# A fused attention and expert kernel: three tiles a turn, logits and turning in 64x64 blocks two tiles back, tile loads in halves

## The reference, cut to what matters

```python
def _attn_ref(q, k, v):
    scores = scale * np.matmul(q, k.transpose(0, 1, 3, 2))
    gamma = 1.0 - 2.0 ** (-5.0 - np.arange(H, dtype=np.float32))
    rel = pos[:, None] - pos[None, :]
    Dmat = np.where(rel >= 0, gamma[:, None, None] ** rel[None, :, :], 0.0)
    return np.matmul(scores * Dmat[None, :, :, :], v)

def _moe_ref(x, phi, w1, w2):
    logits = x @ phi
    d = softmax of logits over the tokens (axis 0)
    slot_input = d.T @ x
    for e in range(E):
        slot_out[e] = np.maximum(slot_input[e] @ w1[e], 0.0) @ w2[e]
    c = softmax of logits over the slots (axis 1)
    return c @ slot_out

def _moe2_ref(x, w1, w2, w3, w_out):
    return ((x @ w1) * (x @ w2) @ w3) @ w_out
```

## Time and profile before

| | |
|---|---|
| median of 3 runs | 394.13 us (391.75 to 395.69) |
| the profiled execution | 394.4 us, span 392.6 us |
| PE busy | 358.9 us, 91% of the span |
| DVE, ACT, POOL busy | 43%, 32%, 41% |
| DMA | 104.77 MB, mean 267 GB/s |
| the tile loop | to about 166 us |

### The profile page before, as it was taken

The page is one execution under the profiler, slowest core; times in us unless marked ns, Lnnn a source line. Parts: engine busy times, 40 slices in busy tenths (PEclk is TensorE's granted clock), DMA queues, the critical chain, the costliest instruction groups (busy, mean ns, idle before and its releaser), DMA issues. The chain is left out here.

```text
span 392.6 us, 16090 instructions
## 1 busy us (share of the span) xinstructions
PE 358.9 (91%) x7123; PEld 278.2 (71%) x7123; DVE 167.5 (43%) x329; ACT 125.2 (32%) x275; POOL 161.9 (41%) x155
## 2 busy tenths in 40 slices
PE   2683987898999999999999999899999999999996
PEld 1573876777878887774656555468878888888885
DVE  1321454556757765573013000699853323233320
ACT  1000121321433342222324220532734444434442
POOL 2521222322443542133546451298954554554530
PEclk9856799999999999999999999999999999999999
DMA  7898499897887886879999996057226655556222
GB/s 262 351 387 341 149 398 426 337 374 250 312 308 240 313 310 231 314 294 411 427 425 427 425 428 273 0 92 237 76 88 228 230 189 188 190 179 235 114 107 107
DMA packets 25914, 104.77 MB, mean 267 GB/s; under 512 B 2660, under 2 KB 5284, under 8 KB 16164
## 3 DMA queue, kind: packets, MB, share of 16 engines
q1 hardware_dynamic: 25892, 104.47, 71.1%
HBM read 94.14 MB, written 10.32 MB: 266 GB/s over the span
## 5 line engine op out<-in xcount | busy, mean ns | idle before, releaser
L561 POOL TENSOR_TENSOR pkg_sb<-pkg_sb,const_sb 128x512 f32<-128x512 f32 x36 | 37.5, 1042 | 106.4 <-DMA pkg_sb<-in_tiles 106.4
L623 POOL TENSOR_TENSOR feat<-c_sb 128x512 f32<-128x512 f32 x45 | 56.9, 1275 | 46.2 <-PE psum L991 44.3
L991 PE MATMUL psum<-m_hi,feat_hi 128*128 128x512 f32 x144 | 56.1, 390 | 0.3 <-DVE m_lo L1480 0.3
L991 PE MATMUL psum<-m_lo,feat_hi 128*128 128x512 f32 x144 | 56.0, 389 | 0.0
L991 PE MATMUL psum<-m_hi,feat_lo 128*128 128x512 f32 x144 | 56.0, 389 | 0.0
L428 DVE TENSOR_TENSOR feat_lo<-feat,feat_hi 128x512 fp32r<-128x512 f32 x34 | 27.2, 801 | 62.2 <-ACT feat_hi L1149 61.0
L1249 DVE TENSOR_TENSOR x_t<-psum,x_decay 128x512 f32<-128x512 f32 x36 | 24.9, 691 | 40.9 <-PE psum L693 40.9
L1007 ACT COPY x_nat<-psum 128x512 f32<-128x512 f32 x36 | 21.1, 586 | 65.8 <-PE psum L705 65.8
L648 PE MATMUL psum<-pkg_sb 64*64 64x64 f32 x1152 | 26.9, 234 | 16.2 <-POOL pkg_sb L561 7.3
L693 PE MATMUL psum<-weights_t,pkg_sb 64*64 64x64 f32 x1152 | 35.3, 238 | 5.7 <-issue 5.5
L1149 ACT CAST feat_hi<-feat 128x512 fp32r<-128x512 f32 x45 | 27.9, 623 | 39.0 <-POOL feat L623 39.0
(11 more groups left out here) (138 smaller groups left out, 569.0 us busy)
## 6 DMA issues: line engine op xcount, KB each, us to landing
pkg_sb<-in_tiles SPq DMA_DIRECT2D x34, 1024.0 KB, 4.9
unit_a<-in_units SPq DMA_DIRECT2D x16, 1024.0 KB, 13.8
c_sb<-c_rows SPq DMA_DIRECT2D x45, 256.0 KB
unit_x<-in_units SPq DMA_DIRECT2D x9, 1024.0 KB, 14.1
out<-out_sb SPq DMA_DIRECT2D x36, 256.0 KB, 2.0
fold_raw<-in_fold SPq DMA_DIRECT2D x6, 1024.0 KB, 9.3
unit_y<-in_units SPq DMA_DIRECT2D x5, 1024.0 KB, 12.3
unit_n<-in_units SPq DMA_DIRECT2D x4, 1024.0 KB, 12.2
```

What stands on the lines that cost most here:

```text
L561: nc.gpsimd.tensor_tensor(v_nat(n).rearrange("p (h d) -> p h d", h=HEADS), v_nat(n).rearrange("p (h d) -> p h d", h=HEADS), decay.unsqueez ...
L623: nc.gpsimd.tensor_tensor(feat[:, k, :], c_sb[:, s, x, :], c_sb[:, s, y, :], ALU.mult).then_inc(feat_ready, 1)
L991: last = mm(psum[:, OUT + b, :], x, y, start=(at == 0 and m == 0), stop=(at == 4 and m == 2))
```

## The change

The loop now has three steps in its body and twelve turns. The parts:

- Tiles load in halves: turned k and q (`load_q_k`), plain k and v (`load_k_v`). The ring has three places. A q half is asked for when `through_states` has used the place (`q_used`), a v half when `update` has. POOL writes scaled v to `v_sb`, in three places of its own, and passes on that the q half is there (`pass_q_k`).
- The fold loads go behind tiles 4 to 7; of the first units two go out with no wait.
- Logits and turning take `x_t` in 64x64 blocks as the stationary side; the turning is a matmul with the identity. The two heads of a pair give separate sums of the logits in two banks, which DVE adds (`add_parts`) and turns. Both are of tile n - 2, and share two banks: logits wait until the turned tile before is copied (`x_copied`), turning waits until the logits are (`logits_copied`).
- The order in a step: logits of n - 2, update of n + 1, turning of n - 2, states, first pass, a dispatch where due, scores of n + 1, second pass. `weights_t` has one place, `x_t` three, `state_sb` six (so `states_used` goes).
- `shift_combine` and `divide_combine` of the first three groups go to POOL.
- Behind the loop, a logits and a turning of tile 34 and of tile 35 stand in turn with fold work.

```diff
-SLOTS_IN = 4
-STATES_IN = 4
+SLOTS_IN = 3
+STATES_IN = 6
...
-FOLD_AT = (10, 11, 14, 15)
+FOLD_AT = (4, 5, 6, 7)
...
+        v_sb = place("v_sb", [P, SLOTS_IN, D])
+        weights_t = place("weights_t", [P, 2, D // 2])
+        x_t = place("x_t", [P, SLOTS_IN, PAIRS, P])
...
+            def load_q_k(n):
 
                 if n >= SLOTS_IN:
 
-                    sp.wait_ge(out_ready, QUARTERS * (n - SLOTS_IN + 1))
-                sp.dma_start(tile_sb(n), pkg[n].rearrange("(p c) -> p c", p=P)).then_inc(tile_loaded[place_of(n)], 16)
+                    sp.wait_ge(q_used, QUARTERS * (n - SLOTS_IN + 1))
+                sp.dma_start(tile_sb(n)[:, 0:2 * D], pkg[n].rearrange("(p c) -> p c", p=P)[:, 0:2 * D]
+                             ).then_inc(q_k_loaded[place_of(n)], 16)
+
+            def load_k_v(n):
+
+                if n >= SLOTS_IN:
+
+                    for i in range(2):
+                        sp.wait_ge(update_ready[i], 2 * (n - SLOTS_IN + 1))
+                sp.dma_start(tile_sb(n)[:, 2 * D:4 * D], pkg[n].rearrange("(p c) -> p c", p=P)[:, 2 * D:4 * D]
+                             ).then_inc(k_v_loaded[place_of(n)], 16)
...
+            load_q_k(0)
+            load_k_v(0)
+            load_k_v(1)
+            load_q_k(1)
...
+            load_k_v(2)
+            load_q_k(2)
             load_first_unit(0)
+            load_first_unit(1)
+            load_k_v(SLOTS_IN)
+            load_first_unit(2)
             for n in range(SLOTS_IN, NTILES):
-                load_tile(n)
-                if n < SLOTS_IN + 2:
-                    load_first_unit(2 * n - 7)
-                    load_first_unit(2 * n - 6)
-                elif n == 8:
+                if n < NTILES - 1:
+                    load_k_v(n + 1)
+                load_q_k(n)
+                if n == SLOTS_IN:
+                    load_first_unit(3)
+                    load_first_unit(4)
+                elif n == SLOTS_IN + 1:
                     load_first_unit(5)
-                elif n in FOLD_AT:
+                if n in FOLD_AT:
...
-                    sp.wait_ge(out_ready, QUARTERS * (NTILES - 3 + (u - 6)))
+                    sp.wait_ge(out_ready, QUARTERS * (NTILES - 2 + (u - 6)))
...
+                pool.wait_ge(k_v_loaded[place_of(n)], (n // SLOTS_IN + 1) * 16)
+                if n >= SLOTS_IN:
+
+                    pool.wait_ge(out_ready, QUARTERS * (n - SLOTS_IN + 1))
                 decay = const_sb[:, C_VDECAY + HEADS * t:C_VDECAY + HEADS * (t + 1)]
                 nc.gpsimd.tensor_tensor(v_nat(n).rearrange("p (h d) -> p h d", h=HEADS),
-                                        v_nat(n).rearrange("p (h d) -> p h d", h=HEADS),
+                                        v_raw(n).rearrange("p (h d) -> p h d", h=HEADS),
                                         decay.unsqueeze(2).to_broadcast([P, HEADS, HD]),
                                         ALU.mult).then_inc(v_ready, 1)
+
+            def pass_q_k(n):
+
+                pool.wait_ge(q_k_loaded[place_of(n)], (n // SLOTS_IN + 1) * 16)
+                pool.sem_inc(q_k_ready, 1)
...
+            pass_q_k(0)
             for n in range(NTILES):
                 scale_v(n)
+                if n > 1:
+                    pass_q_k(n - 1)
                 if 1 <= n <= SEAM:
                     later_decay(n)
+                if n >= TILES + 2:
+                    g, t = divmod(n - 2, TILES)
+                    if t == 3:
+                        shift_combine(nc.gpsimd, pool, g - 1)
+                    if t == 8:
+                        divide_combine(nc.gpsimd, pool, g - 1)
...
+            def turn_x(r, consumes=True):
                 for a in range(PAIRS):
-                    last = nc.tensor.transpose(psum[:, X_NAT, P * a:P * (a + 1)], x_t[:, r % 2, a, :], ident)
-                last.then_inc(x_turned, 1)
-
-            def logits(r):
+                    for odd in range(2):
+                        rows = slice(HD * odd, HD * (odd + 1))
+                        for half in range(2):
+                            cols = slice(HD * half, HD * (half + 1))
+                            last = mm(psum[cols, X_NAT + odd, HD * a:HD * (a + 1)], x_t[rows, r, a, cols],
+                                      ident[rows, rows], start=True, stop=True)
+                            if (a, odd, half) == (0, 0, 0) and consumes:
+                                last.then_inc(logits_copied, -1)
+                            if a == PAIRS - 1:
+                                last.then_inc(x_turned, 1)
...
+            def logits(r, consumes=True):
                 for a in range(PAIRS):
-                    for j in range(SUBS):
-                        last = mm(psum[SLOTS * j:SLOTS * (j + 1), RAW, 0:SLOTS], phi_sb[:, a, :],
-                                  x_t[:, r % 2, a, SLOTS * j:SLOTS * (j + 1)],
-                                  start=(a == 0), stop=(a == PAIRS - 1))
-                        if a == PAIRS - 1:
-                            last.then_inc(logits_ready, 1)
+                    for odd in range(2):
+                        rows = slice(HD * odd, HD * (odd + 1))
+                        for half in range(2):
+                            cols = slice(HD * half, HD * (half + 1))
+                            last = mm(psum[cols, X_NAT + odd, LOGITS_AT:LOGITS_AT + SLOTS], x_t[rows, r, a, cols],
+                                      phi_sb[rows, a, :], start=(a == 0), stop=(a == PAIRS - 1))
+                            if (a, odd, half) == (0, 0, 0) and consumes:
+                                last.then_inc(x_copied, -1)
+                            if a == PAIRS - 1:
+                                last.then_inc(logits_ready, 1)
...
+                two_before, after = [(r + m) % SLOTS_IN for m in (SLOTS_IN - 2, 1)]
+
+                def next_update():
+                    pe.wait_ge(v_ready, 1)
+                    update(after)
+
+                def next_scores():
+                    pe.wait_ge(q_k_ready, 1)
+                    scores(after)
+
+                def earlier_logits():
+                    pe.wait_ge(x_copied, 1)
+                    logits(two_before)
+
+                def earlier_turn():
+                    pe.wait_ge(logits_copied, 1)
+                    turn_x(two_before)
...
+
+                if r == SLOTS_IN - 1:
+                    earlier_logits()
+                else:
+                    with pe.If(i > 0):
+                        earlier_logits()
+
+                pe.wait_ge(states_ready, 1)
                 if r < SLOTS_IN - 1:
-                    next_scores(after)
+                    next_update()
                 else:
                     with pe.If(i < NTILES // SLOTS_IN - 1):
-                        next_scores(after)
+                        next_update()
+                if r == SLOTS_IN - 1:
+                    earlier_turn()
+                else:
+                    with pe.If(i > 0):
+                        earlier_turn()
+
+                pe.wait_ge(x_t_ready, 1)
+                through_states(r)
+                pe.wait_ge(weights_ready, 1)
+                through_scores(r, 0)
                 for g in range(GROUPS - 1):
                     if dispatched_at(g) % SLOTS_IN == r:
                         with pe.If(i == dispatched_at(g) // SLOTS_IN):
                             dispatch(g)
-                if r > 1:
-                    logits(two_before)
+                if r < SLOTS_IN - 1:
+                    next_scores()
                 else:
-                    with pe.If(i > 0):
-                        logits(two_before)
-
-                pe.wait_ge(x_t_ready, 1)
-                through_states(r)
-                pe.wait_ge(logits_copied, 1)
-                through_scores(r, 0)
-                if r > 0:
-                    turn_x(before)
-                else:
-                    with pe.If(i > 0):
-                        turn_x(before)
+                    with pe.If(i < NTILES // SLOTS_IN - 1):
+                        next_scores()
                 pe.wait_ge(phase_done, QUARTERS)
                 through_scores(r, 1)
...
+            pe.wait_ge(x_copied, 1)
             logits(SLOTS_IN - 2)
             fold(1)
             pe.wait_ge(logits_copied, 1)
+            turn_x(SLOTS_IN - 2)
+            fold(1)
+            pe.wait_ge(x_copied, 1)
             pe.wait_ge(x_t_ready, 1)
             logits(SLOTS_IN - 1)
-            turn_x(SLOTS_IN - 1)
-            fold(5)
+            fold(1)
+            pe.wait_ge(group_copied, 2 * GROUPS)
+            turn_x(SLOTS_IN - 1, False)
+            fold(3)
...
+                act.wait_ge(x_turned, QUARTERS * (n + 1))
+                copy(x_nat[:, n % NAT_RING, :].rearrange("p (a k d) -> p k a d", a=PAIRS, k=2),
+                     psum[:, X_NAT:X_NAT + 2, 0:D // 2].rearrange("p k (a d) -> p k a d", a=PAIRS)
+                     ).then_inc(x_nat_ready if n == NTILES - 1 else
```

(34 more changed lines are left out.)

166 lines of the change are left out of this document (72 added, 94 removed).

## The result

The changed kernel takes 396.75 us (median of 20 runs, 394.78 to 398.77), the kernel before beside it 393.33 us (20 runs, 389.90 to 398.11). The ratio is 1.0097, 95% interval 1.0073 to 1.012: about 1% slower, where 381 us, 3% faster, was forecast. The profiled execution of the changed kernel takes 395.4 us with a span of 393.6, that of before 394.4 with 392.6. So the two profiles differ by 1.0 us and the medians by 3.4; what I read from one profile of each can explain the lost gain of 14 us, but not the last 2.4. The choice of execution is a large part of the gap: the profiled one of before lies 1.1 us over its median, that of the changed kernel 1.4 us under its own. The changed kernel's has a mean granted clock of 1.000; the six of its 20 executions with that value have a median of 395.3, the 14 with less 397.0.

The account below looks back on a forecast made before the run. TensorE is full after the last dispatch, so the tile loop ahead sets the time. Last step at 54 + 28 x 3.17 + 3 x 2.6 = 150.6, 14.9 earlier; 394.4 - 14.9 + 1.7 = 381.2 us, range 372 to 390.

Parts of the forecast that it names:

- The average over the clean step: In the tile loop, turns, branches and DVE's group work add 0.12 us to a clean step, giving 3.17.
- The clean step: One undisturbed pass of the changed tile loop takes 3.05 us, against 3.29 before.
- the upper bound: Logits in the loop cost at most as much as a 64x64 group, 0.46 us; 0.34 was taken.
- ScalarE's chain: Logits, ScalarE's copy, turning, states, first pass, scores in the loop: next second pass 3.02 us after the last.
- The loads: Tile halves asked for earlier end the 7.6 us of waits for tiles between steps 7 and 35.
- Step 7: The loop's pass over tile 7, ended by the start of its `x_t`, ends at 54 us instead of 56.51.
- a queue bound of 52: At the start, 19 x 1.05 MB at 426 GB/s, 46.8 us, with 5.4 for the first, gives 52 us.
- Dispatch: Each of three dispatches in the loop, now ahead of the scores, costs 2.6 us instead of 1.96.
- Tail: Behind the loop, turning, copy, addition and transpose put the last dispatch 1.7 us later.
- The rigid block: From the last dispatch to the end, 223.45 us with PE full, unchanged and moving as a whole.
- no change: Rival, 0.07: PE's holes in the loop become waits for ScalarE, steps stay at 3.41 us; 392 to 395.
- Slower: Rival, 0.08: code stops return in loop turns, 3.39 us each, 418 in all; decides from 1.2 us a turn.

Follow-up runs that it names:

- e13: Kernel before with its third dispatch at tile 32 instead of 31 and 13 places for turned tiles instead of 12: 394.14 us, ratio 1.0022.
- e2: Changed kernel with three more never-true dispatch blocks behind the three dispatch conditions: 402.43 us, ratio 1.0254.
- e10: Changed kernel with three more never-true conditions behind the dispatch conditions, each holding one matmul instead of a dispatch: 403.2 us, ratio 1.0269.
- e4: Changed kernel with the turning of x as four 128x128 transposes again, at its new place: 396.55 us, ratio 1.0115.
- e9: e7 with the four early fold loads cut into 16 quarters and both turnings behind the loop as four 128x128 transposes: 388.63 us, ratio 0.9897.
- e7: Changed kernel with its three dispatch conditions inside one more condition, true in 4 of 12 turns: 395.4 us, ratio 1.006.
- e1: Changed kernel with the three dispatch conditions behind the scores instead of ahead of them: 398.8 us, ratio 1.0151.
- e3: Changed kernel with first units and fold loads where they were before the change (folds behind tiles 10, 11, 14, 15): 396.85 us, ratio 1.0102.
- e6: Changed kernel with dispatch conditions and dispatch moved between update and turning, and copy_sums ahead of copy_x on ScalarE: 401.13 us, ratio 1.0218.
- e8: Changed kernel with dispatch conditions between update and turning, nested as in e7, and fold loads behind tiles 8, 10, 12, 14: 400.13 us, ratio 1.0174.
- e5: Kernel before with each of its three dispatch conditions standing three times, the added copies never true: 555.39 us, ratio 1.4159.
- e12: Kernel before with its four early fold loads cut into 16 quarters, two behind tiles 6 and 7, one behind each of 8 to 19: 392.7 us, ratio 0.9985.

## Why the prediction was wrong

Its own sum, term by term, in the profile: last dispatch predicted at 54 + 88.8 (28 steps) + 7.8 (dispatches) + 5.46 + 1.7, and measured 14.4 later.

- **The average over the clean step, wrong, 7.6 us: the main failure.** The step that failed is "Scaled by 4/3 for the turns, 0.12 goes to 0.12 to 0.16". Measured are 3.50 - 3.11 = 0.39, so 0.27 x 28 = 7.6 us. Of the 0.39, 0.24 are the skips (3.84 - 3.11, every third step) and 0.15 the turn. I had counted blocks ("nine in three steps where it had seven in four") and scaled an average that was small because each dispatch condition stood alone where the first is nearly free (e13). The change put three in a row in a place with no cover: 0.68 (row at 124.77), and 0.26 for each added one by e2 and e10. The turn of the loop comes to 0.45 (3.56 against 3.11), where it was 0.33 before (3.61 against 3.28), and comes every third step.
- **The clean step, nearly right, 1.7 us.** 3.11 instead of 3.05. Logits take 0.45, the upper bound. The Trainium skill's rule ("TensorEngine Tiling (Array Packing)", section Performance Considerations), that few columns cost about as much as 60, agrees with this: 32 columns took as long as the 64 of the other groups. But the logits of before, also with 32, took 0.38 with their changeover, and no run parts the columns from the wider stationary side, so that the cause of the 0.45 stays open. ScalarE's chain hid part of it: its copy starts 0.78 after the logits, TensorE turns 0.15 after it ends (122.91), and the turning takes 0.48 for 0.46. e4 shows the new turning worth 0.21 in that step, where I gave it 0.13.
- **The loads, right from step 8 on.** The 7.6 us of waits between steps 8 and 35 went, which is more than the 5.2 that the stretch gained: the rest of it became 2.4 us longer.
- **Step 7, wrong, 5.1 us.** I took 54, between a queue bound of 52 and 56.5, and the answer lay outside on the far side, at 59.05. Up to step 5 the changed kernel is 1.0 us ahead of before; steps 6 and 7 then take 10.07 where before's take 6.56. Of these 3.5 us, 2.7 are the late q halves (against 3.56 and 3.84 for such steps), behind the folds put with tiles 4 to 7; e9, with the folds in quarters, has `x_t` of tile 7 3.0 earlier than e7. The stops of the first pass, 13.6 for 11.2 us, gave nothing back. So the gain of 2.5 us that I had put at the start had no row behind it. I reckoned the queue at 426 GB/s from the start; the first of the 40 slices of the page's bandwidth row (9.8 us) shows 248, and the next three 403 to 413. The bound says when all bytes are there and not which tile comes late.
- **Dispatch, too dear, -1.9 us.** Its step is 1.83 longer than its neighbours of r = 1, and the next by 0.14, 1.97 in all, not 2.6. That this equals the 1.96 of before is chance: the neighbours pay 0.68 for three skips, while in a step with a dispatch only two blocks are skipped, and those behind the dispatch cost nothing (e2). Against a step without skips, 3.84 - 0.68 = 3.16, it costs 2.5 and 0.14, and the 2.6 was right for what it meant.
- **Tail, wrong, 2.2 us.** Without a stop it is 7.3 to 7.7 (e2, e4, e9, e10), 1.8 to 2.3 over before, for 1.7 forecast; the stop in the turning of tile 35 is 1.5 to 1.8 long (after, e1, e3, e6, e7, e8), and the lower clock behind it adds 1.5 in e3, e6 and e7. That it is a stop for code is my reading of "issue"; no run shows the fetch. I had looked for code stops in the loop's first turn and, as a rival, in later turns, but not behind its end, where the change puts 56 more matmul records into the two turnings.
- **The rigid block, right.** From the last dispatch to the span's end it is 221.4 to 221.9 us in every run but e5, where it was not read.

Sum: +7.6 +1.7 +5.1 -1.9 +2.2 = 14.7, for 14.4 measured; the rest is mostly that 10 of the 28 steps are of the short kind, so that their mean is 3.49. Of the rivals, "no change" gave 392 to 395 and came nearest in time, but for the wrong reason: it had ScalarE's chain at 3.41, and where nothing is skipped the chain gives 3.11. "Slower" named the code and a price from 1.2 us a turn; what came was 0.45 for a turn and 0.68 for the skips, 1.1 a turn in all, with no sign of a fetch: the instruction queue moved 14 packets as before. The runs do not show what sets whether the tail stops: e2 and e10 have the same code behind the loop as e1 and stop not.

## What to carry to other kernels

Before moving work in a loop on TensorE, list the conditions of each step and what stands around them: a skipped block cost about 0.25 us whatever its length, three in one place three times that. What hid it here was a long group of matmuls ahead of it (up to five blocks behind a dispatch of 2.07 us), and, for a reason not shown, the place behind the update for one block; a short wait for data hid almost nothing. Nesting rare ones inside one condition takes back all but one. When an average is to be scaled, take the pitch by place in the loop's body first: 3.11, 3.56 and 3.84 said at once what the mean of 3.50 hid. A load between tiles should be smaller than what a step leaves free on the queue (an estimated 0.9 us here): whole ones of 1 MB cost waits of up to 2.3 us, early and late, while quarters cost next to none in e9. With tiles loaded whole, quarters gained nothing (e12).

## What was not expected of the hardware

- A loop can grow too long for TensorE at one blow: between 1,456 and 1,744 load and matmul records in its body the time went from 393 to 555 us (e5), with 87 instruction packets for 14.
- A skipped block costs 0.23 to 0.27 us on TensorE, with 1 matmul in it or 12, and neither 32 records of 64x64 ahead of it (e1) nor 0.2 us of waiting for data (e6, 0.06 covered) hides it. The 24 records of a dispatch hide five (e2: 0.36 to the scores, as with none).
- TensorE can stop behind a loop for 1.5 to 1.8 us with no data wait, in the middle of a group. In three of six such profiles the granted clock then fell to 0.50 for some 3 us (e3, e6, e7), in the other three it stayed at 1.00.
